# Norms of the first five head pairs by matmul from squared columns, and the fifth pair's turns moved forward

## The chip, the cores and the metric

The kernel runs on one core of one Trainium2 chip. The metric is the device time of one execution in microseconds (us). The kernel before took 959.82 us, the median of three runs (959.8, 959.82 and 961.99). Engines are named as in the profile: PE is TensorE (PEld its weight loads), DVE is VectorE, ACT is ScalarE, POOL is GpSimd, SP is SyncE, whose queue issues nearly all DMAs.

## What is computed

Linear attention with random features, then two feed-forward layers on its output. Inputs q, k, v are of 4 batches, 8 heads, 576 tokens and head size 64; omega is 128 x 64.

```
proj = x_scaled @ omega.T                     # x is q or k, scale = 64 ** -0.25
sq   = sum(x_scaled * x_scaled, -1) / 2       # the "half norm" of each row
phi  = exp(proj - sq - max(proj - sq)) / sqrt(128)
kv   = phi(k).T @ v ;  z = sum over tokens of phi(k)
x    = phi(q) @ kv / (phi(q) @ z + 1e-6)      # 2304 tokens x 512
x    = (h * clip(h + 3, 0, 6) / 6) @ w_out    with h = x @ w_in      (512 -> 2048 -> 512)
out  = (h * sigmoid(1.702 * h)) @ w_out2      with h = x @ w_in2
```

## The kernel before, in words

Heads are worked in 16 pairs; a pair's two heads lie in the two halves of the 128 partitions. For each of q and k a pair has a transposed copy (`cols`, 128 x 576), from which PE makes the projections, and a row copy (`rows`, 128 x 9 groups x 64), which serves for nothing but the half norms: squares of the rows, summed over 64. A pair goes through the units q, k and tail (projection on PE, row maxima and two small bias operations on DVE, exponentials on ACT), turn0 and turn1 (PE transposes phi(q), ACT copies it out), kv (PE, then three DVE copies, `keep`), and nd0 and nd1 (numerators and denominators on PE, ACT copies the denominators out with `denominators` or `quotient_part`, DVE takes reciprocals of 1.94 us and multiplies, `normalise`).

The first LEAD = 5 pairs (0 to 4) form a lead phase that runs before the feed-forward work. They alternate between two sets of buffers, a and b. For pair 0 the row squares are made by ACT and summed by one DVE reduction; for pairs 1 to 4 ACT squares, POOL folds 64 to 16 columns in two additions and DVE reduces those (L779); from pair 5 on POOL squares too (`square_rows`, four operations, L362, L364, L350, L352).

After the lead phase the loop over n = 0 to 159 runs the hidden blocks: `hidden(n)` (12 matmuls, L521 to L523: high x high, high x low, low x high part of a split product), gate on ACT, product on DVE (`gated_block`), high part on ACT (`high`), low part on DVE (`low`), and `output(n)` (12 matmuls, L542 to L544). `hidden(0)` is begun inside the lead phase, a quarter of its contraction at a time, as soon as the quarter's high part (`x_hi`, ACT, L662) and low part (`x_lo`, DVE, L840) are there. Between the blocks lie slots g = 2n (behind hidden(n)) and g = 2n + 1 (behind output(n - 1)), into which the units of the other pairs are put, one unit a slot; pair 4's turns, kv, nd0 and nd1 stand at slots 0 to 4, and pair 5 starts with q at slot 5.

Every engine executes its own list in the order written; waits are on semaphore counts. So an instruction that waits holds up all that is behind it on that engine, and this holds for SP too: its list before the loop has, for each of the pairs 2 to 4, row loads, weight loads, the values of the former pair (three DMAs, which wait for kv of the pair two earlier, `kv_done`) and then the pair's two column loads. At the loop's start SP issues one more block of weights when POOL has made low parts (`w_ready`) and then k rows of pair 5 (slot 1); POOL works on them at slot 1, and DVE's reduction of them, `norms(LEAD, KK)`, stands at the end of the iteration n = 1 of its list.

## Time and profile before

| | |
|---|---|
| median of the runs | 959.82 us |
| the profiled execution's own time | 959.88 us |
| its span in the trace | 957.7 us |
| PE busy | 933.1 us (97%) |
| DVE busy | 403.5 us (42%) |
| ACT busy | 383.7 us (40%) |
| POOL busy | 167.1 us (17%) |
| DMA | 45.98 MB, mean 48 GB/s |

The busy times are sums over the whole span. The first 58 us hold the lead phase, in which no engine is always busy; from some 62 us on PE is busy nearly all the time. The granted clock of PE is shown as a share of full speed.

### The profile page before, as it was taken

The page shows a single profiled execution, that of the slowest core. Times are in us where ns is not written, and L with a number is a line of the kernel's source. Part 1 is how long each engine was busy: PE and PEld are TensorE (multiplying, and loading weights), DVE is VectorE, ACT ScalarE, POOL GpSimd, SP SyncE. Part 2 cuts the span into 40 slices and gives each one's busy share as a digit, 9 for nine tenths or more (in the row PEclk, how much of TensorE's full clock was granted, in tenths as well). Part 3 has the DMA queues.
Part 4 walks back from the last instruction along what each step waited for, and adds up shares of the span by engine and source line. Part 5 has one row for each costly group of instructions (what it writes and reads, how often), then busy time and mean ns, then how long its engine had stood idle before and what let it go on. Part 6 is the DMA issues. An engine that isn't in the chain of part 4 may idle for free.

```text
span 957.7 us, 12877 instructions
## 1 busy us (share of the span) xinstructions
PE 933.1 (97%) x5072; PEld 776.9 (81%) x5072; DVE 403.5 (42%) x710; ACT 383.7 (40%) x876; POOL 167.1 (17%) x178
## 2 busy tenths in 40 slices
PE   6879999999999999999999999999999999999998
PEld 5557888788887888888889978888888888888898
DVE  4976545754446544452223342233224222322322
ACT  5665665644446444442225652222223222322322
POOL 3325546212212121000003840000000000000000
PEclk9999999999999999999999999999999999999999
DMA  8513443121212111010002620001001000100010
GB/s 247 156 36 114 140 128 95 49 58 30 62 39 62 39 49 50 1 45 1 1 1 65 182 64 1 0 1 45 1 1 45 0 1 1 44 1 1 7 39 23
DMA packets 40732, 45.98 MB, mean 48 GB/s; under 512 B 21601, under 2 KB 22241, under 8 KB 40673
## 3 DMA queue, kind: packets, MB, share of 16 engines
q1 hardware_dynamic: 38112, 44.51, 15.3%
q10 hardware_dynamic: 2560, 0.66, 0.3%
q8 instruction: 40, 0.66, 0.3%
q14 instruction: 20, 0.16, 0.1%
HBM read 40.44 MB, written 4.72 MB: 47 GB/s over the span
## 4 chain that ended last, share of the span: by engine, by line
PE 91%; DVE 4%; ACT 1%; DMA 1%; issue 1%; POOL 1%; SPq 0%; DVEq 0%; ACTq 0%
PE acc L542 14%; PE acc L543 13%; PE acc L544 13%; PE hid L521 10%; PE hid L523 10%; PE hid L522 10%; PE att L522 3%; PE att L521 3%; PE att L523 3%; PE att L435 2%; PE att L464 2%; PE att L491 2%; PE att L448 1%; DVE k_phi L824 1%; DMA X<-k_n 1%
## 5 line engine op out<-in xcount | busy, mean ns | idle before, releaser
L542 PE MATMUL acc<-g_hi,w_out_hi 128*128 128x512 f32 (+1 forms) x640 | 241.8, 378 | 1.0 <-DVE g_lo L855 0.6
L543 PE MATMUL acc<-g_lo,w_out_hi 128*128 128x512 f32 (+1 forms) x640 | 235.9, 369 | 0.0
L544 PE MATMUL acc<-g_hi,w_out_lo 128*128 128x512 f32 (+1 forms) x640 | 235.7, 368 | 0.0
L521 PE MATMUL hid<-x_hi,w_in_hi 128*128 128x512 f32 (+1 forms) x480 | 184.0, 383 | 5.1 <-DVE x_lo L840 5.1
L523 PE MATMUL hid<-x_hi,w_in_lo 128*128 128x512 f32 (+1 forms) x480 | 177.8, 370 | 0.0
L522 PE MATMUL hid<-x_lo,w_in_hi 128*128 128x512 f32 (+1 forms) x480 | 177.3, 369 | 0.0
L855 DVE TENSOR_TENSOR g_lo<-R,g_hi 128x512 fp32r<-128x512 f32 (+1 forms) x160 | 105.6, 660 | 91.0 <-ACT g_hi L679 90.8
L542 PEld LDWEIGHTS acc<-g_hi,w_out_hi 128*128 128x128 f32 x640 | 120.8, 189 | 23.1 <-issue 2.5
L544 PEld LDWEIGHTS acc<-g_hi,w_out_lo 128*128 128x128 f32 x640 | 120.7, 189 | 20.5
L543 PEld LDWEIGHTS acc<-g_lo,w_out_hi 128*128 128x128 f32 x640 | 120.8, 189 | 19.0
L679 ACT ACTIVATE g_hi<-R 128x512 fp32r<-128x512 f32 (+1 forms) x160 | 94.7, 592 | 86.0 <-DVE R L850 53.1
L521 PEld LDWEIGHTS hid<-x_hi,w_in_hi 128*128 128x128 f32 x480 | 90.8, 189 | 23.2 <-issue 5.1
L848 DVE SCALAR_TENSOR_TENSOR R<-R,hid 128x512 f32<-128x512 f32 (+1 forms) x80 | 50.6, 632 | 134.8 <-ACT R L670 134.8
L523 PEld LDWEIGHTS hid<-x_hi,w_in_lo 128*128 128x128 f32 x480 | 90.7, 189 | 15.9
L522 PEld LDWEIGHTS hid<-x_lo,w_in_hi 128*128 128x128 f32 x480 | 90.9, 189 | 14.5
L670 ACT ACTIVATE R<-hid 128x512 f32<-128x512 f32 (+1 forms) x80 | 44.6, 558 | 107.3 <-PE hid L523 107.3
L850 DVE TENSOR_TENSOR R<-R,hid 128x512 f32<-128x512 f32 (+1 forms) x40 | 25.4, 635 | 114.1 <-ACT R L672 114.1
L850 DVE TENSOR_TENSOR R<-R,att 128x512 f32<-128x512 f32 (+1 forms) x40 | 25.4, 635 | 113.0 <-ACT R L672 113.0
L824 DVE RECIPROCAL k_phi<-k_phi 128x288 f32<-128x288 f32 x28 | 54.5, 1948 | 38.3 <-ACT k_phi L628 38.3
L672 ACT ACTIVATE R<-att 128x512 f32<-128x512 f32 (+1 forms) x40 | 22.2, 555 | 117.0 <-PE att L523 116.8
L672 ACT ACTIVATE R<-hid 128x512 f32<-128x512 f32 (+1 forms) x40 | 22.2, 555 | 116.6 <-PE hid L523 116.5
L522 PE MATMUL att<-x_lo,w_in_hi 128*128 128x512 f32 (+1 forms) x160 | 58.9, 368 | 0.0
(121 smaller groups left out, 1029.8 us busy)
## 6 DMA issues: line engine op xcount, KB each, us to landing
X<-w_in SPq DMA_DIRECT2D x16, 256.0 KB, 2.6
X<-w_out SPq DMA_DIRECT2D x16, 256.0 KB, 2.9
out_t<-X SPq DMA_DIRECT2D x16, 256.0 KB, 2.3
q_cols<-q_t SPq DMA_DIRECT2D x14, 288.0 KB, 3.7
rows<-q_n SPq DMA_DIRECT2D x14, 288.0 KB, 3.0
k_cols<-k_t SPq DMA_DIRECT2D x14, 288.0 KB, 4.0
v_rows<-v_n SPq DMA_DIRECT2D x13, 256.0 KB, 3.4
rows<-k_n SPq DMA_DIRECT2D x11, 288.0 KB, 2.9
```

The costliest lines, as they stand in the source:

```text
L521: nc.tensor.matmul(bank, w_hi[0][:, at], x_hi[:, k, 0:t], start=(k == 0), stop=False)
L522: nc.tensor.matmul(bank, w_hi[0][:, at], x_lo[:, k, 0:t], start=False, stop=False)
L523: last = nc.tensor.matmul(bank, w_lo[0][:, at], x_hi[:, k, 0:t], start=False, stop=(k == KC - 1))
L542: nc.tensor.matmul(bank, w_hi[1][:, at], g_hi[:, g, 0:t], start=(s == 0), stop=False)
L543: nc.tensor.matmul(bank, w_hi[1][:, at], g_lo[:, g, 0:t], start=False, stop=False)
L544: last = nc.tensor.matmul(bank, w_lo[1][:, at], g_hi[:, g, 0:t], start=False, stop=(s == J - 1))
L670: nc.scalar.activation(R[:, 0:t], h, ACT.Relu, bias=3.0).then_inc(gate_ready, 1)
L679: nc.scalar.activation(g_hi[:, n % G_SLOTS, 0:t], R[:, 0:t], ACT.Copy).then_inc(g_hi_ready, 1)
L824: nc.vector.reciprocal(d, d).then_inc(recip_done, 1)
L848: nc.vector.scalar_tensor_tensor(out=r, in0=r, scalar=6.0, in1=h, op0=ALU.min, op1=ALU.mult).then_inc(gated, 1)
L850: nc.vector.tensor_tensor(r, r, h, ALU.mult).then_inc(gated, 1)
L855: nc.vector.tensor_tensor(g_lo[:, n % G_SLOTS, 0:t], R[:, 0:t], g_hi[:, n % G_SLOTS, 0:t].bitcast(F32), ALU.subtract).then_inc(g_ready, 1)
```

## The change

The row copies of pairs 0 to 4 are not loaded any more. ACT squares the columns of q and of k instead (`square_cols`, 128 x 576 each, into two buffers of their own), and PE sums them over the partitions: `norm(a, kind)`, four matmuls with a 128 x 128 block of squares as the stationary operand and a 128 x 2 block of ones as the moving one, and two small ones for the tail. DVE copies the sums out of PSUM (`take_norms`). Since ACT needs the columns as soon as it squares them, its list now has `square_cols` of pair a + 3 behind the first denominators of pair a, for a = 0 and 1; on PE both norms of pair a + 2 stand between `key_values(a)` and `numerator(a, 0)`.

POOL's folds for pairs 1 to 4 are gone. POOL splits three weight blocks ahead of the loop where it split two, and makes the first three low parts of x (`early_low`) in place of DVE. The values of pairs 0 and 1 are loaded from SP's queue where ACT's issued them. Pair 4's two turns and its tail projection now stand between the third and the fourth quarter of hidden(0); hidden(1) goes into another PSUM bank; pair 4's kv is at slot 3 (where it was at slot 2), and both nd0 and nd1 at slot 4. In every hidden block the low-weight product comes ahead of the low-x product.

```diff
-    EARLY_J = 2
+    EARLY_J = 3
...
-            return hid if n < L2 or n % 2 == 0 else att[0]
+            return att[0] if n == 1 or n > L2 and n % 2 else hid
+        def x_lows_to(c, k):
+            return c * KC + k + 1 - (KC - 1)
...
         def slot_units(g):
-            units = []
-            for a in range(LEAD - 1, PAIRS) if g >= 0 else ():
+            units = [(LEAD - 1, u) for u in {3: ("kv",), 4: ("nd0", "nd1")}.get(g, ())]
+            for a in range(LEAD, PAIRS) if g >= 0 else ():
                 at = g - FIRST_SLOT - SLOTS_A_PAIR * (a - LEAD)
                 if 0 <= at < SLOTS_A_PAIR:
-                    if a == LEAD - 1 and at == 3:
-                        units.append((a, "tail"))
                     units.append((a, UNITS[at]))
             return units
...
             def cols(a, kind):
                 if before_in_set(a) >= 0:
                     sp.wait_ge(proj_done, 3 * before_in_set(a) + 3)
+                if 0 <= before_in_set(a) < LEAD:
+                    sp.wait_ge(squared, 2 * before_in_set(a) + 2)
...
             for a in (0, 1):
-                for kind in (KQ, KK):
-                    cols(a, kind)
-                    rows_of(a, kind)
+                cols(a, KQ)
+                cols(a, KK)
+            values(0)
+            values(1)
             for a in (2, 3, 4):
-                rows_of(a, KQ)
-                rows_of(a, KK)
                 weights(a - 2)
                 if a > 2:
                     values(a - 1)
                 cols(a, KQ)
                 cols(a, KK)
             weights(3)
+            rows_of(LEAD, KQ)
             values(4)
-            rows_of(LEAD, KQ)
+            weights(4)
             cols(LEAD, KQ)
             cols(LEAD, KK)
...
+            def early_low(k):
+                pool.wait_ge(x_hi_ready, k + 1)
+                t = SIZES[0]
+                nc.gpsimd.tensor_tensor(x_lo[:, k, 0:t], x_at(k, 0, t), x_hi[:, k, 0:t].bitcast(F32), ALU.subtract).then_inc(x_early, 1)
...
-            for a in (1, 2, 3, 4):
-                sum_rows(a, KQ)
-                sum_rows(a, KK)
-                if a > 1 and a - 2 < EARLY_J:
-                    early_weights(a - 2)
+            for j in range(EARLY_J):
+                early_weights(j)
             square_rows(LEAD, KQ)
+            for k in range(KC - 1):
+                early_low(k)
...
+            def norm(a, kind):
+                pe.wait_ge(squared, 2 * a + kind + 1)
+                if a >= 2:
+                    pe.wait_ge(turned_out, 2 * (a - 2) + 2)
+                elif 2 * a + kind > 0:
+                    pe.wait_ge(norms_ready, 2 * a + kind)
+                x, sums = col_squares[kind], norm_sums(a)[:, kind, :]
+                for t in range(ST):
+                    nc.tensor.matmul(sums[:, 0:2 * ST].rearrange("p (h t) -> p t h", h=2)[:, t, :], x[:, t * P:(t + 1) * P],
+                                     head_ones[:], start=True, stop=True)
+                for h in range(2):
+                    rows_h = slice(h * D, (h + 1) * D)
+                    last = nc.tensor.matmul(sums[rows_h, 2 * ST:GROUPS], x[rows_h, ST * P:S], head_ones[rows_h, h:h + 1],
+                                            start=True, stop=True)
+                last.then_inc(norm_done, 1)
...
-                else:
-                    pe.wait_ge(den_ready, dens_to(a, 0, 0))
+                elif by_columns(a):
+                    pe.wait_ge(den_ready, dens_to(a, 0))
+                if by_columns(a) and half == 0 and a == 0:
+                    pe.wait_ge(norms_ready, 4)
+                if by_columns(a) and half == 1 and a + 2 < LEAD:
+                    pe.wait_ge(norms_ready, norms_to(a + 2, KK))
                 tokens = slice(half * HALF, (half + 1) * HALF)
                 if by_columns(a):
@@ -487,7 +514,11 @@
                 else:
                     if half == 1:
                         pe.wait_ge(tails_out, a + 1)
+                    elif a == LEAD - 1:
+                        pe.wait_ge(gated, 2)
                     for h in range(2):
+                        if half == 1 and h == 1:
+                            pe.wait_ge(den_ready, dens_to(a, 0, 0))
...
-                if 0 < n <= L2:
+                if n == 1:
+                    pe.wait_ge(turned_out, 2 * (LEAD - 1) + 2)
+                elif n == 2 or n > L2 + 1:
+                    pe.wait_ge(gated, n - 1)
+                elif n > 0:
                     pe.wait_ge(gated, n)
-                elif n > L2 + 1:
-                    pe.wait_ge(gated, n - 1)
                 bank = hid_bank(n)[:, 0:t]
                 for k in blocks_k:
                     if s == 0:
-                        pe.wait_ge(x_ready, c * KC + k + 1)
+                        pe.wait_ge(x_hi_ready, c * KC + k + 1)
                     at = slice(s * 512 + k * P, s * 512 + (k + 1) * P)
                     nc.tensor.matmul(bank, w_hi[0][:, at], x_hi[:, k, 0:t], start=(k == 0), stop=False)
-                    nc.tensor.matmul(bank, w_hi[0][:, at], x_lo[:, k, 0:t], start=False, stop=False)
-                    last = nc.tensor.matmul(bank, w_lo[0][:, at], x_hi[:, k, 0:t], start=False, stop=(k == KC - 1))
+                    nc.tensor.matmul(bank, w_lo[0][:, at], x_hi[:, k, 0:t], start=False, stop=False)
+                    if n == 0 and k < KC - 1:
+                        pe.wait_ge(x_early, k + 1)
+                    elif s == 0:
+                        pe.wait_ge(x_ready, x_lows_to(c, k))
+                    last = nc.tensor.matmul(bank, w_hi[0][:, at], x_lo[:, k, 0:t], start=False, stop=(k == KC - 1))
...
-            for u in ("q", "k", "tail"):
-                projection(0, u)
+            projection(0, "q")
+            pe.wait_ge(ones_set, 4)
+            norm(0, KQ)
+            projection(0, "k")
+            norm(0, KK)
+            projection(0, "tail")
             pe.wait_ge(ident_ready, 1)
             pe.wait_ge(v_fixed, 10)
             turn(0, 0)
+            projection(1, "q")
+            norm(1, KQ)
             turn(0, 1)
-            projection(1, "q")
             projection(1, "k")
+            norm(1, KK)
             for a in range(LEAD - 1):
                 if a + 1 < LEAD - 1:
                     projection(a + 1, "tail")
                 key_values(a)
+                if a + 2 < LEAD:
+                    norm(a + 2, KQ)
+                    norm(a + 2, KK)
                 if a + 1 == LEAD - 1:
                     hidden(0, (0,))
                 numerator(a, 0)
@@ -567,13 +613,15 @@
                 if a + 2 < LEAD:
                     projection(a + 2, "q")
                 numerator(a, 1)
-                if a + 1 < LEAD - 1:
+                if a + 2 < LEAD:
                     turn(a + 1, 0)
-                if a + 2 < LEAD:
                     projection(a + 2, "k")
-                if a + 1 < LEAD - 1:
                     turn(a + 1, 1)
-            hidden(0, (2, 3))
+            hidden(0, (2,))
+            turn(LEAD - 1, 0)
+            turn(LEAD - 1, 1)
+            projection(LEAD - 1, "tail")
+            hidden(0, (3,))
...
+            def square_cols(a, kind):
+                act.wait_ge(load_cols[in_set_b(a)][kind], 16 * loads_in_set(a))
+                if a > 0:
+                    act.wait_ge(norm_done, 2 * (a - 1) + kind + 1)
+                nc.scalar.activation(col_squares[kind][:], xt_of(a, kind), ACT.Square, scale=SCALE * 0.5 ** 0.5).then_inc(squared, 1)
...
-            square_rows(0)
-            square_rows(1)
+            square_cols(0, KQ)
+            square_cols(0, KK)
             exps_of(0, "q")
+            square_cols(1, KQ)
             exps_of(0, "k")
             turned_head(0, 0)
+            square_cols(1, KK)
             turned_head(0, 1)
             exps_of(0, "tail")
-            square_rows(2)
+            square_cols(2, KQ)
+            square_cols(2, KK)
             for a in range(LEAD - 2):
                 exps_of(a + 1, "q")
                 denominators(a, 0)
+                if a + 3 < LEAD:
+                    square_cols(a + 3, KQ)
+                    square_cols(a + 3, KK)
                 exps(a + 1, "k", 0)
                 denominators(a, 1)
                 exps(a + 1, "k", 1)
                 exps_of(a + 1, "tail")
                 turned_head(a + 1, 0)
-                if a + 3 < LEAD:
-                    square_rows(a + 3)
-                else:
+                turned_head(a + 1, 1)
+                if a + 3 == LEAD:
                     act.wait_ge(x_written, 2 * (PPB - 2))
                     split(0, (0, 1))
-                turned_head(a + 1, 1)
-            act.wait_ge(x_written, 2 * (PPB - 1))
-            split(0, (2,))
             denominators(LEAD - 2, 0)
             exps(LEAD - 1, "q", 0)
             denominators(LEAD - 2, 1)
             exps(LEAD - 1, "q", 1)
+            act.wait_ge(x_written, 2 * (PPB - 1))
+            split(0, (2,))
+            turned_head(LEAD - 1, 0)
+            turned_head(LEAD - 1, 1)
...
+                    exps_of(LEAD - 1, "tail")
...
+            def take_norms(a, kinds):
+                dve.wait_ge(norm_done, 2 * a + kinds[-1] + 1)
                 if a >= 2:
                     dve.wait_ge(bias_ready, 3 * (a - 2) + 3)
-                nc.vector.reduce_sum(half_norm[:, a % 2, kind, :], x, AX_X).then_inc(norms_ready, 1)
-            def maxima(a, u):
-                dve.wait_ge(proj_done, units_to(a, u))
+                at = slice(kinds[0], kinds[-1] + 1)
+                nc.vector.tensor_copy(half_norm[:, a % 2, at, :], norm_sums(a)[:, at, :]).then_inc(norms_ready, 1)
...
             for u, kind in (("q", KQ), ("k", KK)):
                 maxima(0, u)
-                norms(0, kind)
+                take_norms(0, (kind,))
                 biases(0, u)
             statistics(0, "tail")
-            norms(1, KQ)
+            take_norms(1, (KQ,))
             statistics(1, "q")
-            norms(1, KK)
+            take_norms(1, (KK,))
             for a in range(LEAD - 2):
                 keep(a)
-                norms(a + 2, KQ)
                 statistics(a + 1, "k")
+                take_norms(a + 2, (KQ, KK))
                 statistics(a + 1, "tail")
                 normalise(a, 0)
                 normalise(a, 1)
                 if a + 2 < LEAD - 1:
                     statistics(a + 2, "q")
-                else:
-                    split(0, (0, 1))
-                norms(a + 2, KK)
             keep(LEAD - 2)
             statistics(LEAD - 1, "q")
             normalise(LEAD - 2, 0)
             normalise(LEAD - 2, 1)
-            split(0, (2, 3))
-            statistics(LEAD - 1, "k")
+            dve.wait_ge(proj_done, units_to(LEAD - 1, "k"))
+            maximum(LEAD - 1, "k", 0)
+            split(0, (KC - 1,))
+            maximum(LEAD - 1, "k", 1)
+            biases(LEAD - 1, "k")
+            statistics(LEAD - 1, "tail")
...
+                    elif what == "kv":
+                        keep(a)
...
-                    attend(a, what)
+                    if what == "nd0":
+                        normalise(a, 0)
+                    else:
+                        attend(a, what)
```

## Rows read from the trace of the kernel before

**Rows 1.** The head of the page: span and instructions.

```profile
span 957.7 us, 12877 instructions
```

**Rows 2.** Windows; columns: stretch, its length, PE busy, granted clock, DMA, GB/s.

```profile
62.00:64.00 2.00, 2.00 (x5) 0.50 0.00 0
64.00:66.00 2.00, 2.00 (x17) 0.83 0.00 0
...
170.00:958.00 788.00, 782.93 (x4108) 658.01 (x4106) 296.63 (x510) 282.94 (x609) 85.57 (x87) 1.00 0.10 30
```

**Rows 3.** Timeline of PE in the lead phase: start, us, engine, line, operation, records.

```profile
19.09 1.90 PE L464 MATMUL att<-v_rows,k_phi 128*128 128x65 f32 x16
...
30.18 1.90 PE L464 MATMUL att<-v_rows_b,k_phi_b 128*128 128x65 f32 x16
...
35.25 2.08 PE L435 MATMUL acc<-omega,X 64*128 64x128 f32 x16
...
39.63 1.16 PE L435 MATMUL acc<-omega,X 64*128 64x128 f32 x16 [0.41 <-ACT k_phi L611]
...
42.29 1.90 PE L464 MATMUL att<-v_rows,k_phi 128*128 128x65 f32 x16
44.77 1.19 PE L484 MATMUL att<-q_phi,state 128*64 128x288 f32 x8 [0.58 <-DVE state L818]
...
51.37 1.90 PE L464 MATMUL att<-v_rows_b,k_phi_b 128*128 128x65 f32 x16
```

**Rows 4.** Timeline of SP's queue: the issues behind the first kv.

```profile
21.31 0.65 SPq L289 DMA_DIRECT2D v_rows<-v_n  x1
...
23.70 0.58 SPq L274 DMA_DIRECT2D X<-q_t  x1
```

**Rows 5.** DMA issues; the last column is us from issue to landing.

```profile
X<-k_t SPq DMA_DIRECT2D x1, 288.0 KB, 3.5
...
k_cols<-k_t SPq DMA_DIRECT2D x1, 288.0 KB, 3.1
```

**Rows 6.** Timeline of ACT.

```profile
12.21 2.16 ACT L611 ACTIVATE q_phi<-acc,bias 128x128 f32<-128x128 f32 x8
...
24.90 1.14 ACT L611 ACTIVATE k_phi_b<-acc,bias 128x128 f32<-128x128 f32 x4 [2.18 <-DVE bias L799]
...
40.33 0.74 ACT L594 ACTIVATE rows<-rows 128x576 f32<-128x576 f32 x1
...
68.76 0.71 ACT L647 ACTIVATE w_in_hi<-X 128x512 fp32r<-128x512 f32 x1
```

**Rows 7.** The chain that ended last, 69 to 76 us: start, us, what.

```profile
69.55 1.27 POOL w_in_lo L371
...
72.47 2.94 DMA rows<-k_n
```

**Rows 8.** Timeline of DVE behind hidden(1).

```profile
71.61 0.28 DVE L817 COPY state<-att 128x128 f32<-128x128 f32 x1
...
78.86 0.30 DVE L779 TENSOR_REDUCE half_norm<-rows 128x9 f32<-128x144 f32 x1 [5.78 <-POOL rows L352]
```

**Rows 9.** Timeline of PE from the lead phase's end on.

```profile
61.83 0.77 PE L521 MATMUL hid<-x_hi,w_in_hi 128*128 128x512 f32 x1 [4.21 <-DVE x_lo L840]
...
66.23 0.47 PE L521 MATMUL hid<-x_hi,w_in_hi 128*128 128x512 f32 x1
...
78.42 0.61 PE L542 MATMUL acc<-g_hi,w_out_hi 128*128 128x512 f32 x1
...
90.01 1.16 PE L435 MATMUL att<-omega,k_cols 64*128 64x128 f32 x16 [0.91 <-ACT q_phi L611]
```

**Rows 10.** The chain that ended last: numerators of one slot.

```profile
105.40 0.97 PE att L491 x4
```

**Rows 11.** Timeline of POOL and DVE at 84 us.

```profile
84.75 1.29 POOL L371 TENSOR_TENSOR w_out_lo<-X,w_out_hi 128x512 fp32r<-128x512 f32 x1
...
84.93 1.13 DVE L796 SCALAR_TENSOR_TENSOR h_max<-row_max,half_norm 128x8 f32<-128x8 f32 x1
```

111 lines of the change are left out of this document (49 added, 62 removed).

## The prediction

> **What bounds the kernel now.** I read the page, then windows of 2 us over the first 84 us, then the timelines of all engines there, SP's queue and the landings of its transfers, and last the chain of waits. The span is 957.7 us [rows 1], the execution 959.88 us, so 2.18 us lie around the span; the median of the runs is 959.82 us, so what I add to the execution's own time is added to the median too (within 0.1 us). From 170 us on PE is busy 782.93 of 788.00 us [rows 2]: there nothing can be gained or lost but PE's own work, which this change leaves alone. So the time follows when PE gets through the lead phase and how whole its work is in the first few slots. In the lead phase each pair ends in a kv, whose last group ends at 20.99, 32.08, 44.19 and 53.27 us (start plus duration of the four L464 rows [rows 3]): steps of 11.1, 12.1 and 9.1 us. Then PE waits 4.21 us for low parts of x, runs at 1.2 GHz (granted 0.50) and from 66.23 us runs full [rows 2, 9]. output(1) starts at 78.42 us, 25.15 us behind the last lead kv; I use it as the mark at which both kernels have done the same work on PE.
>
> **Part 1, the front, up to kv of pair 0.** The exponentials of q start at 12.21 us [rows 6], since ACT issues value DMAs and squares four row tiles first. Now they need only projection, PE norm, the copy and the biases: projection from 5.5 us, norm behind it, start at about 10.2 us, 2.0 us sooner. But PE now has four norms before kv(0). A norm is four matmuls with 128 x 128 stationary blocks, two records each; the nearest row is L464 (same stationary size, 65 columns), 1.90 us for 16 records [rows 3], 0.12 us a record. So 8 records are 0.95 us, and with the two small ones 1.15 us; bounds 0.95 (the small ones free) and 1.45 us (all 12 records at full price). Four of them are 4.6 us, of which the first two lie in PE's old wait for those exponentials and the rest eats the gain; the squares of k of pair 1 also stand behind exponentials on ACT. kv(0) ends at 20.7 us, **-0.3 us**; bounds -1 and +1.3 (one POOL operation in the way of a bias, below).
>
> The Trainium skill, "TensorE: Matmul & The Clock Gate", section "LDWEIGHTS (loading the stationary operand)", says that the load takes the time of the columns whatever the number of rows. By that rule the projections' price (64 rows, 128 columns, 1.16 us for 16 records, 0.07 each [rows 3]) would hold for the norms, 0.6 us each; the L464 row speaks against it, since there 128 rows cost 0.12. By the rule the sum would be 1 to 2 us smaller.
>
> **Part 2, kv(0) to kv(1) and kv(1) to kv(2).** Here I expect the loss. ACT's list has the squares of pair a + 3 behind the first denominators of pair a and ahead of exps(a + 1, k, 0), denominators(a, 1) and everything after. They need pair a + 3's columns. SP issues these behind the three value DMAs that wait for kv(a): after kv(0) at 20.99 the first goes out at 21.31 and q's columns at 23.70 us [rows 4], 2.7 us behind kv's end; k's follow 0.6 later, 3.3 behind. They land 3.5 us after issue in that place, 3.1 where less is under way [rows 5]; with the rows' transfers gone I take 3.1: 6.4 us behind kv. A square is 0.74 us [rows 6]: 7.1 us. In the kernel before the projection that uses these columns ran much later, at 35.25 us [rows 3], so the transfer was hidden; now the cover is gone. exps(1, k, 0) started at 24.90 us [rows 6], and from there to kv(1)'s end are 7.2 us: denominators, second half of the exponentials, projection of pair 2's k (which waits for the bank), turn, tail, kv, one after another on ACT and PE. So kv(1) comes 7.1 + 7.2 = 14.3 us behind kv(0) and not 11.1. Before it PE idles about 3 us, and after 4.21 us of idling it was granted 0.50 for a while [rows 2, 9]; the same projection took 2.08 us at 35.25 and 1.16 at 39.63 [rows 3]. I add that 0.9: 15.2, a loss of **+4.1 us**; the bounds are 0.9 less and, with the slower landing, 0.4 more.
>
> For pair 1 all is the same: 15.2 in place of 12.1, **+3.1 us** (bounds +2.2 and +4.0). The two norms of 2.3 us between kv and numerator are covered in both steps by the wait for the squares, and so is DVE's shorter list.
>
> **Part 3, kv(2) to kv(3).** There are no squares. But numerator(2, 0) started 0.58 us behind kv (44.19 to 44.77) [rows 3]; now two norms stand before it, 2.3 us, and the copy of state lies beside them. PE goes on from there to the denominators, the exponentials that wait behind them, and the next projection: 1.8 us later, less 0.3 of old gaps: **+1.5 us** (bounds 0, if DVE with its 1.94 us reciprocals is the bound anyway, and +2.3). The step becomes 10.6 us.
>
> **Part 4, from kv(3) to output(1).** Times count from kv(3)'s end. DVE: keep, maxima and biases of q of pair 4, 2.4 us; ACT: two halves of exponentials with denominators between, then x_hi(2) to 5.7; POOL's low part, at the 1.27 us of its low parts [rows 7], to 7.1. PE: end of the third quarter, turns, tail, to 8.9; ACT copies the turns, x_hi(3) to 9.65; x_lo(3) on DVE 0.7, hidden(0) done at 10.7. hidden(1) needs no gate now and runs to 13.5. Meanwhile DVE has half of the maxima of k, biases, tail and the norm of pair 5 (2.1 us) ahead of gated_block(0), then high and low: output(0) at 14.5, a new wait of 1.0 us. Up to here this saves 1 to 2 us.
>
> But ACT's high part of weight block 3 starts behind exponentials at 15.5, and in the kernel before it started at 68.76 [rows 6], 15.5 behind kv(3) too. On it hangs a chain that the change does not shorten: POOL's low part from 69.55, k rows of pair 5 issued at 72.47 with 2.94 us on the way [rows 7], four POOL operations, DVE's norm of 0.30 us at 78.86 [rows 8]; 10.4 us in all. Before, the copy of kv(4) into state, 71.61 [rows 8], stood ahead of that norm in DVE's list, since kv was at slot 2. Now kv is at slot 3, and DVE's list has norms(5, k) at the end of n = 1 and keep(4) at the start of n = 2: keep(4) waits for a row transfer it has nothing to do with. State is ready at 15.5 + 10.4 + 0.5 = 26.4. PE has output(0) from 14.5 (2.8 us), kv (2.1) and hidden(2) (2.8), is done with them at 22.2 and waits 4.2 us at nd0. Four numerators, at 0.97 us for two [rows 10], put output(1) at 28.4 in place of 25.15: **+3.2 us** (bounds -1.0 with keep not held up, +4.5). After a wait of 4 us PE is granted 0.50 for 2 us and 0.83 for 2 more [rows 2], which costs 1.0 + 0.3: **+1.3 us** (bounds 0 and 2). The 0.91 us wait of pair 5's second projection for exponentials [rows 9] goes, since PE is late and they aren't: **-0.9 us**.
>
> What costs nothing: low parts on POOL (it has lost the folds), the third early weight block (its load is issued long before), values from SP's queue (they land before kv(0)). The rest of the loop keeps its waits.
>
> Where POOL and DVE meet: h_max, a DVE operation on two small SBUF operands, normally 0.17 us, took 1.13 us at 84.93 and ended with POOL's operation of 84.75 [rows 11]. The Trainium skill, "SBUF — State Buffer", section "Who interferes with whom", has the rule: a DVE instruction with two SBUF inputs and a GpSimd one that reads SBUF exclude each other. By that rule, with which the trace agrees, the folds' removal gives DVE back some 3 us in the lead phase, and the three weight blocks in one piece can take as much at other places; since DVE isn't what ends last in parts 2 and 3, I give it nothing.
>
> **Sum.** -0.3 + 4.1 + 3.1 + 1.5 + 3.2 + 1.3 - 0.9 = +12.0 us; 959.88 + 12.0 = **971.9 us**.
>
> **Rivals.** (A) The columns land in time (less traffic, or the squares don't end last) and only keep(4) is late. Then all three steps are PE chains of 10.6 us: -0.3 - 0.5 - 1.5 + 1.5 + 3.2 + 1.3 - 0.9 = +2.8, **962.7 us**. For it: less is loaded. Against: 2.7 us of the delay is issue order on SP, which traffic doesn't touch. (B) The squares are late but keep(4) isn't (k rows of pair 5 come sooner): 8.4 - 1.0 - 0.9 = +6.5, **966.4 us**. Against it: three serial resources of before stand unchanged in its chain. (C) Faster: both stalls are absent. The mechanism is DVE's relief: reciprocals and maxima bound the lead phase, its list loses reductions, three x_lo of 0.7 and waits for POOL, and PE's norms lie in gaps. -0.3 - 0.5 - 1.5 + 0 - 1.0 - 0.9 = -4.2, **955.7 us**. It decides from the point at which columns of pair 3 land within some 4 us of kv(0) and k rows of pair 5 are summed before hidden(2) ends. For it: DVE's wait times in the lead phase are short; against it: rows 4 and 5 give 6.4 us. (D) Losses only in part, cancelled by A's gains: no change, about 960. (E) Every idle stretch brings 1.2 GHz over more of PE's work than I count, and landings are slow as SP issues in bunches: **976 us**.
>
> **Chances.** Forecast 0.50, A 0.13, B 0.15, C 0.10, D 0.05, E 0.07. A measurement of this kernel can tell about 0.3%, 2.9 us, from no change. Faster 0.10 (C), same 0.07 (D and a part of A), slower 0.83. The range goes from A's side at 961.5 to E's at 976: it leaves out C, D and a tail above, together under 2 in 10. The forecast's own range is 968 to 975.
>
> **What would show it.** ACT: squares of pairs 3 and 4 preceded by idle time that a DMA of columns ends, 2 to 3 us each. Last kv groups ending near 20.7, 35.9, 51.1 and 61.7 us. PE: a wait of about 4 us at nd0 of pair 4, released by the copy into state, and that copy right behind DVE's norm of pair 5 and POOL's last fold. output(1) near 90 us. Granted 0.50 behind each of the long waits. The forecast is wrong if kv(1) ends before 33 us, or if state of pair 4 is copied as soon as its kv ends.

## The result, and the profile after

The changed kernel takes 984.56 us (median of 4 runs, 980.68 to 986.91), the kernel before on the same chip 959.81 us: a ratio of 1.025 with an interval of 1.0211 to 1.0289. It is 24.8 us slower. The forecast had the sign right and the size wrong: 971.9 us, with a range that ended at 976. The profiled execution took 986.91 us, with a span of 985.0 where [rows 1] has 957.7, so the span grew by 27.3.

The head of the page of the kernel after, and its first line of busy times:

```profile
span 985.0 us, 13117 instructions
PE 961.1 (98%) x5192; PEld 799.8 (81%) x5192; DVE 398.2 (40%) x708; ACT 383.6 (39%) x874; POOL 161.4 (16%) x167
```

The same marks as in [rows 3] and [rows 9], on the timeline of PE of the kernel after (start, us, engine, line, operation, records). L487 is kv, L522 the numerators, L579 the first matmul of output(1):

```profile
27.07 3.52 PE L487 MATMUL att<-v_rows,k_phi 128*128 128x65 f32 x16
...
43.90 1.90 PE L487 MATMUL att<-v_rows_b,k_phi_b 128*128 128x65 f32 x16
...
57.63 1.90 PE L487 MATMUL att<-v_rows,k_phi 128*128 128x65 f32 x16
...
69.42 1.90 PE L487 MATMUL att<-v_rows_b,k_phi_b 128*128 128x65 f32 x16
...
97.93 4.21 PE L522 MATMUL att<-q_phi,state 128*128 128x288 f32 x8 [4.22 <-DVE state L869]
...
101.53 1.04 PE L579 MATMUL acc<-g_hi,w_out_hi 128*128 128x512 f32 x1
```

Start plus duration of the four kv rows gives 30.59, 45.80, 59.53 and 71.32 us, where before had 20.99, 32.08, 44.19 and 53.27. The table sets each stage against the forecast (us):

| stage | before | forecast | after | after less before |
|---|---|---|---|---|
| start to the end of kv(0) | 20.99 | 20.7 | 30.59 | +9.6 |
| kv(0) to kv(1) | 11.1 | 15.2 | 15.2 | +4.1 |
| kv(1) to kv(2) | 12.1 | 15.2 | 13.7 | +1.6 |
| kv(2) to kv(3) | 9.1 | 10.6 | 11.8 | +2.7 |
| kv(3) to output(1) | 25.15 | 28.4 | 30.2 | +5.1 |

So output(1) starts 23.1 us later (101.53 less 78.42). From the second projection of pair 5 (113.32 less 90.01 us) to the last kv group the delay stays between 23.3 and 23.7 us, and at the boundary of the two layers, at 577 to 589 us, it grows to 26.5 us, which is also the delay of the last matmul. The biggest single item is the first row, which the forecast had at -0.3.

The agreement of the second row is chance. The forecast's 15.2 us there hang on squares that wait for their columns, and in this execution the squares of pair 3, at 36.12 us, waited for none; PE filled the step with norms and numerators at half pace. Those of pair 4 did wait. ACT of the kernel after:

```profile
36.12 0.68 ACT L642 ACTIVATE q_col_squares<-X 128x576 f32<-128x576 f32 x1
...
51.09 0.68 ACT L642 ACTIVATE q_col_squares<-q_cols 128x576 f32<-128x576 f32 x1 [1.96 <-DMA q_cols<-q_t]
```

**The front runs at half pace.** PE in the front, timeline of the kernel after. The sixteen records of the projection (L441) are the same work as L435 in [rows 3], and take 2.08 us at half pace and 1.16 at full:

```profile
5.91 2.08 PE L441 MATMUL acc<-omega,q_cols 64*128 64x128 f32 x16 [5.91 <-DMA omega<-omega_t]
7.92 1.86 PE L454 MATMUL att<-head_ones,q_col_squares 128*128 128x2 f32 x8
...
36.66 2.08 PE L441 MATMUL acc<-omega,q_cols 64*128 64x128 f32 x16
...
41.24 1.16 PE L441 MATMUL acc<-omega,k_cols 64*128 64x128 f32 x16 [0.41 <-ACT k_phi_b L659]
...
45.63 1.00 PE L454 MATMUL att<-head_ones,q_col_squares 128*128 128x2 f32 x8
...
46.77 1.05 PE L454 MATMUL att<-head_ones,k_col_squares 128*128 128x2 f32 x8
```

And the windows of PE of the same kernel there (stretch, its length, PE busy and records, granted clock, DMA share, GB/s):

```profile
6.00:20.00 14.00, 14.00 (x94) 1.00 0.56 157
20.00:39.00 19.00, 19.00 (x114) 1.00 0.25 76
```

The two views contradict each other, and the pace decides: every known group of 5.9 to 38.7 us lasts twice (2.08 for 1.16, 3.52 for 1.90 us) although the windows' clock reads 1.00. That is the lower level, 1.2 GHz. The windows read 1.00 from the start to the first fall, at 48 to 50 us, straight through the rise at 39 us that the durations show; why, no run shows. The other thing to see is that PE is never idle in those 33 us: a busy share of 100% looks like an engine at work and is an engine at half speed. In the kernel before, the first two projections were at half pace too, so were its turns behind the wait of 3.20 us that follows them (eight records at 13.48 us in 2.06 us, where the same eight take 1.03 at full pace), and the group at 15.5 us (L435 x32 in 2.71 us) came up to full.

A norm costs 45.63 to 46.77, 1.14 us, at full pace, just as the forecast priced it (1.15); at half pace it is 7.92 to 10.02, 2.1 us.

**The later falls of the clock.** Windows of PE after the norms of pairs 2 and 3, and around nd0:

```profile
50.00:52.00 2.00, 2.00 (x16) 0.50 0.98 345
...
64.00:66.00 2.00, 2.00 (x14) 0.50 0.27 103
...
98.00:100.00 2.00, 2.00 (x4) 0.50 0.30 93
100.00:102.00 2.00, 2.00 (x6) 0.50 0.64 217
102.00:104.00 2.00, 2.00 (x6) 0.50 0.92 248
```

The first two stand behind two norms each, and there PE was not idle; the last three stand behind the wait of 4.22 us at nd0 and last 6 us, where [rows 2] shows 2 us at 0.50 and 2 at 0.83.

**nd0 of pair 4.** POOL, then DVE, of the kernel after:

```profile
93.81 1.15 POOL L362 TENSOR_TENSOR rows<-rows 128x576 f32<-128x576 f32 x1 [4.11 <-DMA rows<-k_n]
...
96.66 0.49 POOL L368 TENSOR_TENSOR rows<-rows 128x144 f32<-128x144 f32 x1
97.18 0.30 DVE L821 TENSOR_REDUCE half_norm<-rows 128x9 f32<-128x144 f32 x1 [6.94 <-POOL rows L368]
97.40 0.28 DVE L868 COPY state<-att 128x128 f32<-128x128 f32 x1
97.60 0.28 DVE L869 COPY state<-att 128x128 f32<-128x128 f32 x1
```

This is the sequence of part 4 to the letter: row transfer, POOL's folds, DVE's norm of pair 5, and only behind it the two copies of a state whose kv had ended at 90.90 us.

### The profile page after: what moved, and what is told of

The parts are those of the page before. It is cut to its first block, busy times and chain, and to the rows that moved or that the text cites. A ratio compares the mean times of both kernels' runs of the same rounds, so it can differ in the third digit from the quotient of the medians.

```text
span 985.0 us, 13117 instructions
## 1 busy us (share of the span) xinstructions
PE 961.1 (98%) x5192; PEld 799.8 (81%) x5192; DVE 398.2 (40%) x708; ACT 383.6 (39%) x874; POOL 161.4 (16%) x167
## 4 chain that ended last, share of the span: by engine, by line
PE 93%; DMA 2%; ACT 1%; DVE 1%; POOL 1%; issue 1%; SPq 0%; ACTq 0%; DVEq 0%
PE acc L579 13%; PE acc L580 13%; PE acc L581 13%; PE hid L554 10%; PE hid L560 10%; PE hid L555 10%; PE att L554 3%; PE att L560 3%; PE att L555 3%; PE att L487 3%; PE att L522 3%; PE att L441 2%; PE acc L441 2%; PE att L471 1%; PE att L454 1%; PE att L511 1%
## 5 line engine op out<-in xcount | busy, mean ns | idle before, releaser
L579 PE MATMUL acc<-g_hi,w_out_hi 128*128 128x512 f32 (+1 forms) x640 | 242.5, 379 | 2.2 <-DVE g_lo L906 1.3
L554 PE MATMUL hid<-x_hi,w_in_hi 128*128 128x512 f32 (+1 forms) x476 | 181.6, 382 | 3.0 <-ACT x_hi L710 2.4
L555 PE MATMUL hid<-x_hi,w_in_lo 128*128 128x512 f32 (+1 forms) x476 | 175.5, 369 | 0.0
L579 PEld LDWEIGHTS acc<-g_hi,w_out_hi 128*128 128x128 f32 x640 | 121.0, 189 | 24.4 <-issue 3.2
L554 PE MATMUL att<-x_hi,w_in_hi 128*128 128x512 f32 (+1 forms) x164 | 60.5, 369 | 1.1 <-DVE R L901 1.1
```

The costliest lines, as they stand in the source:

```text
L554: nc.tensor.matmul(bank, w_hi[0][:, at], x_hi[:, k, 0:t], start=(k == 0), stop=False)
L555: nc.tensor.matmul(bank, w_lo[0][:, at], x_hi[:, k, 0:t], start=False, stop=False)
L579: nc.tensor.matmul(bank, w_hi[1][:, at], g_hi[:, g, 0:t], start=(s == 0), stop=False)
```

## The experiments

Times are medians, each with its ratio against the kernel before on the same chip (961.1 us for the first four, 960.98 for the next four, 961.19 for the last four). When these were planned, two things were open: what held the clock down (theory: matmuls of few moving columns; rival: only what those matmuls wait for and bring along), and how the rest divides between the columns' transfers, keep(4) and the norms' own time.

**Thin matmuls in the kernel before.** Eight matmuls with 128 x 128 blocks behind kv of pairs 0 to 2, with 2 moving columns, and the same with 64:

```diff
+                extra(a)   # for a < 3: 8 x matmul(three(a)[1][:, 0:N], tile_of(a, KK, h, t), omega2[:, 0:N]); N = 2 or 64
```

> The kernel before, with eight more matmuls (128 x 128 stationary tiles of phi(k), 2 moving columns of omega, results not used) behind kv of pairs 0, 1 and 2; nothing else is changed. Theory N (narrow matmuls pull PE's clock down): each group takes 1.9 us at 2.4 GHz, and the granted clock goes to 0.50 behind it for 3 us or more, where PE was at full clock before; 965 to 972 us in all. Rival L (a narrow matmul costs only its own time, and the changed kernel's loss comes from waits and transfers): the granted clock falls no more often than before, each group delays the numerators by 1.3 us, and the time is 961 to 964 us.

> The same eight matmuls in the same places with 64 moving columns in place of 2. The stationary loads are the same, so each group takes the same 1.9 us. Theory N: the clock stays at full level behind the groups, 961 to 964 us, below the run with 2 columns by 4 us or more. Rival L: the same time as the run with 2 columns, within 1 us. A third way (any PE work that isn't a long matmul counts as idle, whatever its columns): both fall alike and both are at 965 us or more.

With 2 columns 962.49 us (1.001, 0.9998 to 1.0021), with 64 columns 961.5 (1.0, 0.9989 to 1.0011). The difference is 1.0 us: theory N's sizes were missed, and the rival's times were met. In one place theory N's fall can be seen all the same, behind the third group of thin matmuls, in windows of the kernel with 2 columns:

```profile
46.00:48.00 2.00, 2.00 (x19) 0.94 0.71 159
48.00:50.00 2.00, 2.00 (x16) 0.50 0.54 144
```

PE was busy for all of 46 to 50 us and fell to 0.50. With 64 columns nothing fell there. But behind the first two groups nothing fell with 2 columns either, so thin matmuls do not bring a fall each time. (The kernel before has a fall of its own, at 35.25 us in [rows 3], behind a wait of PE; with the extra groups that wait and that fall are gone.) And 1 us is no explanation for 24.8.

**Wider ones in the changed kernel.** The norms' ones 48 columns wide, copies of the same sums:

```diff
-        head_ones = sb("head_ones", [P, 2])
+        head_ones = sb("head_ones", [P, 48])
```

> The changed kernel with the block of ones 48 columns wide in place of 2 (24 of each head), so that a norm matmul has the same stationary loads and moves 24 times the columns; DVE takes one column of each 24 out, in two or three copies in place of one. Theory N: PE is granted full clock in most of the first 40 us, kv(0) ends near 21 to 23 us where it ended at 30.6, and the time is 968 to 974 us, what the prediction had (972). Rival L: no change beyond the extra copies, 984 to 987 us.

984.35 us (1.0228, 1.02 to 1.0257): no gain, as the rival said. The front stays at half pace up to about 40 us. The falls at 50 and 64 us are gone, and what they had covered comes up: the turns of pair 2, which waited 0.95 us in the changed kernel, now wait 2.77 for the exponentials behind the squares (54.45 us). So the first of the later falls cost next to nothing: where PE waits for ACT anyway, half pace eats idle time, and kv(1) to kv(2) takes 14.0 us here against 13.7. The second cost 1.2 us, since kv(2) to kv(3) takes 10.6 here against 11.8.

**keep(4) ahead of the norm.** norms(5, k) behind slot 2's work in DVE's list:

```diff
-                    if g == 2:
+                    if g == 4:
                         norms(LEAD, KK)
```

> The changed kernel with DVE's norm of pair 5's k moved behind the iteration n = 2, so that keep of pair 4 doesn't stand behind it. Prediction's part 4: the wait of 4.2 us at nd0 and the half clock behind it go, 5 to 7 us less than the changed kernel's 984.6: 978 to 980 us. Rival (the wait moves to gated_block(2) or to pair 5's exponentials, since the row sums still come late): 982 to 985 us.

981.46 us (1.0183, 1.0126 to 1.024); the four executions took 970.66, 981.03, 981.88 and 983.3. Each against its own kernel before, that is 4.4 us less than the changed kernel, where 5 to 7 was expected. The wait at nd0 is gone. The execution of 970.66 is the one that the profile caught, and its timeline of PE shows why it stands apart:

```profile
14.08 1.11 PE L471 MATMUL att<-ident,q_phi 128*128 128x128 f32 x4
15.13 1.71 PE L441 MATMUL acc<-omega,X 64*128 64x128 f32 x16
...
18.55 1.16 PE L441 MATMUL acc<-omega,X 64*128 64x128 f32 x16
...
21.72 1.90 PE L487 MATMUL att<-v_rows,k_phi 128*128 128x65 f32 x16
```

Here full pace comes within the group at 15.13 us, not at 39, with the same instructions in front as in the changed kernel. kv(0) ends at 23.6 us and not at 30.6, and the execution is 10.4 us shorter than the lowest of the other three. The length of the slow front thus varies between executions of the same instructions. That the other three had the slow front is likely but not shown, since they weren't traced; shown are the 7.0 us at kv(0).

This trace also gives the front's price when its clock comes up where that of before does: 23.6 us, 2.6 behind before, and outside the forecast's bounds (20.7, at most 1.3 more).

**Norms that move 512 columns.** Each norm's four block matmuls become one with omega stationary and 512 columns of squares moving; the norms are then not the reference's:

```diff
-                for t in range(ST):
-                    nc.tensor.matmul(sums[...][:, t, :], x[:, t * P:(t + 1) * P], head_ones[:], ...)
+                nc.tensor.matmul(bank[:, 0:512], omega2[:], x[:, 0:512], start=True, stop=True)
```

> The changed kernel with the four block matmuls of each norm replaced by one matmul that moves 512 columns of the squares past omega as the stationary tile (0.85 us at 2.4 GHz, about what the four took; the half norms are then not the reference's). The runs so far show that in the changed kernel PE runs at half pace from its first instruction to about 39 us, whether 2 or 48 columns are moved, and that one execution in which it came to full pace at 15.8 us took 970.7. Theory M (the rise to full clock waits for stretches in which PE streams, and weight-load-bound norms in front break them up): full pace is reached by 16 us, kv(0) ends at 20 to 23 us and the time is 968 to 974 us. Rival W (what keeps the clock down is that PE has no pause: steady work at half pace without an idle stretch): as before, kv(0) near 30 us, 981 to 987.

976.92 us (1.0184, 1.0148 to 1.0219), 15.9 above before. PE's timeline of this kernel:

```profile
7.20 1.73 PE L454 MATMUL att<-q_col_squares,omega 128*128 128x512 f32 x2
...
9.06 1.16 PE L441 MATMUL acc<-omega,k_cols 64*128 64x128 f32 x16
10.16 1.13 PE L454 MATMUL att<-k_col_squares,omega 128*128 128x512 f32 x2
...
18.68 1.90 PE L486 MATMUL att<-v_rows,k_phi 128*128 128x65 f32 x16
...
28.60 0.79 PE L470 MATMUL att<-ident,q_phi_b 128*128 128x128 f32 x4 [2.30 <-ACT k_phi L668]
29.63 2.08 PE L441 MATMUL acc<-omega,k_cols 64*128 64x128 f32 x16 [0.24 <-ACT k_phi_b L658]
...
33.52 1.90 PE L486 MATMUL att<-v_rows_b,k_phi_b 128*128 128x65 f32 x16
...
59.80 1.90 PE L486 MATMUL att<-v_rows_b,k_phi_b 128*128 128x65 f32 x16
```

A norm at full pace is about as dear as before (1.13 + 0.28 us overlapping in part, some 1.2 from start to start of what follows, against 1.14 to 1.19), so its own time hardly changed; the pace did. Full pace comes at 9 us, and kv(0) ends at 20.58 us against a forecast of 20.7; the kernel with the same front further down, whose clock came up at 12.39 us, has 22.82, so the closeness is in part luck. The next three steps are 14.8, 15.5 and 10.8 us against 15.2, 15.2 and 10.6, so with the front at full clock the forecast's steps hold. The time itself lies 3 us above theory M's 974, and rival W is out: PE had no pause here between its first matmul and 26 us, and came up at 9 us. The edit changes two things together, the columns moved and the number of stationary blocks loaded (one for four), and doesn't part them. The squares wait for their columns as it said, on ACT:

```profile
25.70 0.68 ACT L641 ACTIVATE q_col_squares<-X 128x576 f32<-128x576 f32 x1 [1.64 <-DMA X<-q_t]
...
41.05 0.68 ACT L641 ACTIVATE q_col_squares<-q_cols 128x576 f32<-128x576 f32 x1 [2.15 <-DMA q_cols<-q_t]
```

**A quarter of the norms' block matmuls.** One in place of four:

```diff
-                for t in range(ST):
-                    nc.tensor.matmul(sums[...][:, t, :], x[:, t * P:(t + 1) * P], head_ones[:], ...)
+                nc.tensor.matmul(sums[:, 0:2 * ST], x[:, 0:P], omega2[:, 0:2 * ST], start=True, stop=True)
```

> The changed kernel with one block matmul for each norm in place of four (9 groups from one, so the half norms are not the reference's): three quarters of the norms' PE time are left out. Theory M: the front has projections nearly back to back, full pace by 12 to 18 us, 964 to 970 us. Rival W: PE still has pauses as before the change, so it too says early full pace; then only the length of the slow stretch against the moving form tells them apart. If full pace comes at 30 us or later even so, both are wrong and the front's order (turns and projections of pair 1 interleaved) is the cause.

975.64 us (1.0151, 1.0131 to 1.0171), 14.7 above before. Still half pace: L441 takes 2.08 us at 6.06, 8.90, 13.74 and 17.62, and full pace comes within the group at 29.16 us. The time is 6 us above theory M's range. Each norm is 1.3 us shorter at half pace (0.8 for 2.1), and kv(0) ends at 25.65. So less thin work shortens the slow front, but doesn't remove it. Where the clock came up is seen on PE of this kernel (L509 are the numerators, 288 moving columns; at full pace 1.19 us):

```profile
27.05 2.19 PE L509 MATMUL att<-q_phi,state 128*64 128x288 f32 x8
29.16 1.77 PE L441 MATMUL acc<-omega,q_cols 64*128 64x128 f32 x16
```

It came within the second of these groups. In all four traces with a slow front the first quicker group lies 2 to 6 us behind the start of the first numerators, wherever those stand: 34.54 and 38.66 us in the changed kernel, 34.58 and 38.71 with 48 columns, 27.05 and 29.16 here, 34.63 and 40.88 with all repairs. So the rise came earlier here as the numerators did, and the run doesn't show that less thin work brings it. The expectation blamed the front's order in this case; no run changed only that.

**The second half of the change, alone.** The kernel before with pair 4's transposes and tail ahead of the first expert block's end and with the new order of slots, without any norm by matmul; then the same with keep first; then with the wait of hidden(81) as it was:

```diff
-                elif n > 0:
+                elif 0 < n <= L2:
                     pe.wait_ge(gated, n)
```

> The kernel before with the second half of the change alone: early low parts on POOL, pair 4's turns and tail inside hidden(0), hidden(1) in another bank, kv at slot 3, nd0 and nd1 at slot 4; norms and product order as before. By the prediction's part 4: hidden(0) earlier, then keep of pair 4 behind the late norm of pair 5's k, +2 to +4 us against before: 962 to 965. Rival: the early turns win more than the late keep loses: 957 to 960.

> The same with DVE's norm of pair 5's k moved behind the iteration n = 2, so that keep isn't held up. If part 4 is right this takes back the wait of some 4 us and the half clock behind it: 957 to 960 us, 3 to 6 us under the run without it, and it beats the kernel before by 1 to 3 us. Rival (PE is full anyway): no more than 1 us between the two.

> The kernel of e8 (kernel before, second half of the change, norm of pair 5's k behind n = 2; 961.9 us) without the new wait of hidden(81). The wait is 1.1 us in e8's trace and a wait of PE there, so 960.5 to 961.2 us, the same as before within what can be measured. If it wins more than 2 us the wait had more behind it; if nothing, x_lo or the gate's product ends last there.

966.67 us (1.0065, 1.005 to 1.008), 961.85 (1.0009, 0.9995 to 1.0024) and 960.72 (0.9994, 0.9981 to 1.0008). The first two lie 1.7 and 1.9 us above what was expected of them, the third within it. The wait at nd0 in the first of the three:

```profile
82.25 3.84 PE L505 MATMUL att<-q_phi,state 128*128 128x288 f32 x8 [3.75 <-DVE state L847]
```

and in the second, where the numerators start with none:

```profile
79.19 2.31 PE L505 MATMUL att<-q_phi,state 128*128 128x288 f32 x8
```

Moving norms(5, k) is worth 4.8 us by the medians. The two traces give 3.75 of wait, and 1.5 from the group itself (3.84 against 2.31), which ran slow behind the wait. The last step is worth 1.1 us, the size of a wait that the change adds without meaning to. The waits of PE from 110 us on in the kernel after (what waited for what: us in total, times, longest):

```profile
PE hid L560 <- DVE x_lo L891: 1.1, 2, 0.6
PE att L554 <- DVE R L901: 1.1, 1, 1.1
```

The second is hidden(81), the second hidden block of the second layer. The condition before was `0 < n <= L2` and then `n > L2 + 1`, which left n = L2 + 1 = 81 without a wait for the gates; the rewritten `elif n > 0` catches it. In the traces PE's waits between 500 and 640 us sum to 1.5 us before, to 2.2 to 3.7 in the changed kernel and the two here with its condition, and to 1.4 to 1.5 in the three kernels that have the old condition back. With the second half repaired in both places the kernel is level with before: that half, by itself, gains nothing that can be measured.

**Columns ahead of values.** The kernel with 512 moving columns, and in SP's list the columns of pair a + 3 ahead of the value transfers:

```diff
                 weights(a - 2)
-                if a > 2:
-                    values(a - 1)
                 cols(a, KQ)
                 cols(a, KK)
+                if a > 2:
+                    values(a - 1)
```

> The kernel of e5 (changed kernel, norms as one moving matmul, full clock from 9 us on, 976.9 us; half norms not the reference's) with SP issuing the columns of pairs 3 and 4 ahead of the values of the former pair in place of behind them. The prediction's part 2 says that the squares end last, because SP's issue order puts the columns 2.7 us behind kv: then the two steps of 14.8 and 15.6 us fall to 11 to 12, PE's waits of 2.3 and 2.8 us at the turns go, and the time is 968 to 971. Rival P (PE's and ACT's own chain, longer by the norms, would be late anyway): steps above 14 us, 975 or more.

970.14 us (1.0092, 1.0072 to 1.0111): 6.8 us less than with the values first. PE and then ACT of this kernel:

```profile
20.92 1.90 PE L486 MATMUL att<-v_rows,k_phi 128*128 128x65 f32 x16
...
28.91 0.63 PE L470 MATMUL att<-ident,q_phi_b 128*128 128x128 f32 x4 [0.38 <-ACT k_phi L668]
...
32.60 1.90 PE L486 MATMUL att<-v_rows_b,k_phi_b 128*128 128x65 f32 x16
...
44.28 1.90 PE L486 MATMUL att<-v_rows,k_phi 128*128 128x65 f32 x16
...
54.96 1.90 PE L486 MATMUL att<-v_rows_b,k_phi_b 128*128 128x65 f32 x16
```

```profile
26.19 0.68 ACT L641 ACTIVATE q_col_squares<-X 128x576 f32<-128x576 f32 x1
```

The squares no longer wait, the turn waits 0.38 us where it waited 2.30, and the steps are 11.7, 11.7 and 10.7 us where they were 14.8, 15.5 and 10.8. Part 2's price of a loss behind SP's list is confirmed where the front runs at full clock: 6.8 us in the time, against 7.2 forecast.

**All three repairs.** The changed kernel with its real norms, columns first, keep first and the old wait; then the same with a 512-column matmul, whose result is not used, ahead of each of the first four norms:

```diff
+                if a < 2:
+                    nc.tensor.matmul(att[1][:, 0:512], omega2[:], x[:, 0:512], start=True, stop=True)
```

> The changed kernel, norms as in it, with three repairs: columns ahead of values on SP, DVE's norm of pair 5's k behind n = 2, and hidden(81) without its new wait for the product of block 80 (1.1 us in the traces of all kernels with the second half of the change). The slow clock in front is left. 984.6 less some 3 (columns; in the slow front the squares were hardly late), less 6 (keep and the half clock behind it), less 1.1: 972 to 976 us. Rival (the repairs are hidden behind the slow front): 978 or more.

> The same with one more matmul ahead of each of the first four norms, which moves 512 columns of squares past omega into the bank that the norm then overwrites; 0.6 to 0.9 us of PE each. Theory S (what brings PE to full pace in front is streaming of columns, so added work makes it faster): full pace by 9 to 10 us, 8 to 11 us less than e10: 963 to 967 us. Rival: the early rise in e5 came from the norms' absence and not from the moved columns: PE stays at half pace past 25 us and the time is 2 to 3 us above e10.

972.87 us (967.04 to 979.33; ratio 1.0101, 1.0054 to 1.0148) and 970.98 (967.62 to 974.52; 1.0102, 1.0069 to 1.0135). The profiled execution of the first, 979.33 us, had half pace to 41 us. With the added matmuls full pace came by 15.3 us, but the clock fell again behind the norms of pairs 2 and 3 (the projections at 31.77 and 46.19 us took 2.08 us each). The difference of 1.9 us lies inside the scatter and settles nothing. The first lies within what was expected of it; the second met neither the theory (full pace by 10 us, 963 to 967) nor its rival (half pace past 25 us). Neither is as fast as before, so no version here beats it.

In the first of the two no square waits any more, and yet its steps are longer than with 512 moving columns. PE of this kernel:

```profile
27.17 3.51 PE L487 MATMUL att<-v_rows,k_phi 128*128 128x65 f32 x16
...
44.27 1.90 PE L487 MATMUL att<-v_rows_b,k_phi_b 128*128 128x65 f32 x16
...
58.30 1.90 PE L487 MATMUL att<-v_rows,k_phi 128*128 128x65 f32 x16
...
71.91 1.90 PE L487 MATMUL att<-v_rows_b,k_phi_b 128*128 128x65 f32 x16
```

The last two steps are 14.0 and 13.6 us, against 11.7 and 10.7 in the kernel with the columns first and 512 moving columns. In both, the numerators and the projection behind the norms ran at half pace (the projections at 50.77 and 65.12 us took 2.08 each). So the later falls are cheap only as long as PE would wait anyway: with the columns in time they cost 2 to 3 us a pair in this execution.

## Why the prediction was wrong, point by point

Differences are each kernel's median less that of the kernel before on its own chip: 24.75 for the change, 15.9 with 512 moving columns, 8.95 with the columns first as well.

- **Part 1, the front: failed, and this is the step that broke the prediction.** It had kv(0) at 20.7 us, "-0.3", with bounds -1 and +1.3. It was 30.59. A norm's price of 1.15 us was right, but it is the price at full clock, taken from a row at 19 us, and apart from one POOL operation the bounds were bounds of that price alone. (The doubt about it, 0.6 us by the projections' row, was idle: in the trace of before one load takes 0.19 us with 128 rows and with 64 alike, and what differs is how closely the records follow each other, 0.12 and 0.07 us.) The four norms stand where PE runs at half pace, and with them that stretch went on to 38.7 us. The kernel with the same order but 512 moving columns had kv(0) at 20.58; this term is 24.75 - 15.9 = 8.8 us of the time. Even with the clock coming up as early as in before, the changed kernel's own norms put kv(0) at 23.6 in the one trace that has it. The hint was in the trace of before: the first projections (1.92 and 2.08 us) ran at half pace, and the forecast counted them without asking what brings the clock up.
- **Part 2, squares behind the columns: the mechanism was right, but in the changed kernel the match of the first step was luck.** The order of issue on SP was as written (kv(0) ended at 30.59, q's columns went out at 32.64 us). But PE was at half pace up to 39 us, the squares of pair 3 waited for nothing, and the 15.2 us of that step are PE's own. In the second step the squares waited 1.96 us, and it took 13.7, since no low clock followed the short wait of PE. With the front at full clock both steps came as written: squares that wait 1.64 and 2.15 us, 14.8 and 15.5 us, and a low clock behind each wait of PE (2.08 us for the projection at 29.63). There the part is worth 15.9 - 8.95 = 7.0 us, forecast 7.2.
- **Part 3, norms between kv and numerator: right at full clock.** 10.8 and 10.7 us with the clock up, forecast 10.6; the 11.8 of the changed kernel holds the fall at 64 us as well, which the forecast didn't have: it let the clock fall behind waits only.
- **Part 4, keep(4): right in mechanism and wait.** 4.2 us forecast, 4.22 measured, released by the copy behind DVE's norm. Undoing it alone gives 4.8 us back, between kernels that differ in nothing else; the forecast's own difference, from +3.2 to its bound of -1.0 and 1.3 for the clock, is 5.5. In the changed kernel the low clock lasts 6 us instead of 4, which is most of why the stage took 30.2. The gain of 1 to 2 us that the part books for the earlier turns doesn't show: with the copy and hidden(81) both repaired, that half is level with before (-0.5 us, -1.8 to +0.8).
- **The 0.91 us of pair 5's second projection: right.** It starts at 113.32 us in the kernel after with no wait.
- **Missing: hidden(81).** "The rest of the loop keeps its waits" was wrong. The diff rewrote the condition, and the one value of n that the old one let through was not checked. 1.1 us as measured directly, 1.3 by differences to before. In the profiled execution the delay grew by 2.8 us at that place.

The terms found are 8.8, 7.0, 4.8 and 1.3, 21.9 of 24.75 us. The 2.8 that are left are the first half's net cost with everything late repaired and 512 moving columns in the norms; kv(3) ended at 56.86 us there, 3.6 behind before, 1.8 of them up to kv(0) and 1.8 in the three steps. That they are the norms is argued, not separated. The sum adds what each repair gave in the order in which they were made; in the slow front the columns alone would give less, as the squares that didn't wait show.

Rival C (faster) needed keep(4) in time and the columns landed: keep(4) was 4.22 us late and the squares of pair 4 waited 1.96 us for theirs. Rival A's world, columns in time and keep late, is the kernel with 512 moving columns and the columns first, and gave +8.95 where A had +2.8: A's sum puts kv(3) at 52.5 us, it ended at 56.86 (kv(0) at 22.82, two steps of 11.7 and not 10.6), and hidden(81) adds its 1.3. Rival E named the right cause, 1.2 GHz over more of PE's work than was counted, and sized it at 4 us: it took it to follow idle stretches, when it came without any.

What stays open is the rule by which the clock comes up in the front. With a 512-column matmul at the start it came up at 9 us in one kernel and at 12 and 15 in two others; with 48 columns it did not; a quarter of the norms left it at half pace to 29; and the one traced execution of the kernel with keep first came up at 15 us on the same instructions as the changed kernel. Each of these is one trace. No run here separates the kind of work from what varies between executions.

## What to carry to other kernels

Price small PE work at both clock levels and ask which holds where it is put: four norms priced at 4.6 us put kv(0) 9.6 us later, since they lay in a slow front and that front stayed slow. A step that agrees with the forecast is no proof either: look whether the wait that it was added up from is there. When an instruction's operand now comes from a transfer or an engine it did not use before, list what stands ahead of it and behind it in that engine's order, since a copy that waits behind another pair's norm costs its whole wait and the clock after it. And when a diff rewrites a guard, run through the values that neither branch took.

## What the runs showed of the hardware that was not expected

- PE stayed at half pace from 5.9 to 38.7 us without one idle microsecond, while the granted clock read 1.00, as it did through the rise at 39 us; a known group's duration (1.16 or 2.08 us for sixteen records) is the reading to trust.
- The length of that slow stretch varies between executions of the same instructions: full pace came at 15 us in one trace and at 39 in another, and kv(0) ended at 23.6 and 30.6 us. The times of the four executions of the first kernel (970.66 against 981.03 to 983.3) fit that. The kernel before doesn't scatter so: over all its runs it took 958.81 to 963.75 us, though in the traces of kernels with its front the clock came up for good anywhere between 16 and 20 us.
- The clock fell to 0.50 behind norms of 2 columns with PE busy throughout (50 to 52, 64 to 66 us), and not with 48 columns. It fell so too in the traces of the kernel with keep first and of both with all repairs, whose norms have 2 columns; in the lead phase of the two kernels with 512 moving columns it fell only behind waits, or not at all.
